# Router logits computed the other way round: the expert vectors as the stationary operand, three token tiles side by side in TensorE's columns

## What is computed

```python
# 1: linear attention, then an RMS norm           -> x [2304, 512]
# 2: dense mixture: out += p[:, e] * (relu(x @ w1[e]) @ w2[e]) for 4 experts
# 3: routed mixture, 8 experts, one for each token
xn = x / (norm(x) + 1e-6);  en = expert_emb / (norm(expert_emb) + 1e-6)
logits = xn @ en.T / tau                        # [2304, 8]
expert_idx = argmax(logits)
gate_w = softmax(logits)[expert_idx]
out[mask_e] = gate_w * (relu(x[mask_e] @ w1[e]) @ w2[e])
```

## Time and profile before

| | us |
|---|---|
| median of 3 runs | 1151.87 |
| runs | 1150.92 to 1154.58 |
| the profiled execution, own time | 1151.53 |
| its span | 1149.9 |
| PE busy | 1125.5 (98%) |
| DVE busy | 728.5 (63%) |
| ACT busy | 455.3 (40%) |
| POOL busy | 655.9 (57%) |

### The profile page before, as it was taken

The page is one execution under the profiler, slowest core; times in us unless marked ns, Lnnn a source line. Parts: engine busy times, 40 slices in busy tenths (PEclk is TensorE's granted clock), DMA queues, the critical chain, the costliest instruction groups (busy, mean ns, idle before and its releaser), DMA issues.

```text
span 1149.9 us, 18699 instructions
## 1 busy us (share of the span) xinstructions
PE 1125.5 (98%) x6206; PEld 992.3 (86%) x6207; DVE 728.5 (63%) x1159; ACT 455.3 (40%) x808; POOL 655.9 (57%) x609
## 2 busy tenths in 40 slices
PE   8999999999999999999999999999999999999996
PEld 8888889999889888998889888998887788888885
DVE  4877888888976788888875878888662222222221
ACT  4773444444434444444434444444222222222220
POOL 1587777799867777899867777777330111111101
PEclk9999999999999999999999999999989999999998
DMA  9955777777512448877612448777369749427960
GB/s 245 268 157 180 267 268 271 278 275 276 199 45 78 142 131 302 289 278 261 216 37 75 137 146 302 279 273 270 144 243 383 273 183 372 153 100 302 374 238 13
DMA packets 102433, 250.87 MB, mean 218 GB/s; under 512 B 8254, under 2 KB 48190, under 8 KB 94171
## 3 DMA queue, kind: packets, MB, share of 16 engines
q1 hardware_dynamic: 97360, 235.18, 59.2%
q0 software_dynamic: 4800, 14.72, 3.7%
q10 hardware_dynamic: 203, 0.05, 0.0%
HBM read 170.99 MB, written 79.98 MB: 218 GB/s over the span
## 4 chain that ended last, share of the span: by engine, by line
PE 82%; DVE 7%; POOL 4%; issue 3%; DMA 2%; ACT 2%; SPq 0%; DVEq 0%; POOLq 0%; ACTq 0%
PE ps L1277 25%; PE ps L1279 25%; PE ps L1278 25%; PE ps L1466 2%; DMA w_raw<-in_moe_w_dram 1%; DVE x_rows L965 1%; POOL w_lo L483 1%; PE ps L1235 1%; PE ps L1432 1%; PE ps L1370 1%; DVE hT_lo L954 1%; PE ps L1205 1%; DVE attn_rows L887 1%; DVE x_ops_lo L978 1%; DVE hT_lo L952 0%
## 5 line engine op out<-in xcount | busy, mean ns | idle before, releaser
L1277 PE MATMUL ps<-x_ops_hi,w_hi 128*128 128x384 f32 x672 | 226.5, 337 | 3.4 <-DVE sum L935 3.2
L1277 PE MATMUL ps<-w_hi,hT_hi 128*128 128x512 f32 x576 | 227.1, 394 | 0.4
L1279 PE MATMUL ps<-x_ops_hi,w_lo 128*128 128x384 f32 x672 | 225.7, 336 | 0.0
L1279 PE MATMUL ps<-w_hi,hT_lo 128*128 128x512 f32 x576 | 225.4, 391 | 0.0
L1278 PE MATMUL ps<-x_ops_lo,w_hi 128*128 128x384 f32 x672 | 225.2, 335 | 0.0
L1278 PE MATMUL ps<-w_lo,hT_hi 128*128 128x512 f32 x576 | 225.0, 391 | 0.0
L965 DVE SCALAR_TENSOR_TENSOR x_rows<-ps,dense_probs,x_rows 128x512 f32<-128x512 f32 x270 | 189.8, 738 | 22.2 <-PE ps L1279 22.2
L608 POOL DMA_INDIRECT out_dram<-y_rows,row_ids x22 | 22.6, 1026 | 237.3 <-DVE y_rows L1168 141.9
L492 POOL TENSOR_TENSOR w_lo<-w_raw,w_hi 128x512 fp32r<-128x512 f32 x96 | 149.5, 1577 | 8.0 <-ACT w_hi L702 8.0
L1158 DVE TENSOR_TENSOR rhT_lo<-ps,rhT_hi 128x512 fp32r<-128x512 f32 x44 | 28.4, 686 | 172.9 <-ACT rhT_hi L826 172.9
L478 POOL TENSOR_TENSOR w_lo<-w_raw,w_hi 128x512 fp32r<-128x512 f32 x48 | 62.2, 1295 | 126.7 <-ACT w_hi L690 126.6
(11 more groups left out here) (198 smaller groups left out, 2006.8 us busy)
## 6 DMA issues: line engine op xcount, KB each, us to landing
w_slots<-split_parts SPq DMA_DIRECT2D x64, 1024.0 KB, 5.6
w_raw<-in_moe_w_dram SPq DMA_DIRECT2D x96, 512.0 KB, 3.5
ahead_raw<-in_moe_w_dram SPq DMA_DIRECT2D x64, 512.0 KB, 6.6
split_parts<-ahead_hi SPq DMA_DIRECT2D x64, 512.0 KB, 4.4
split_parts<-ahead_lo SPq DMA_DIRECT2D x64, 512.0 KB, 5.8
row_tile<-dispatched_rows POOLq DMA_DIRECT2D x20, 257.0 KB, 5.8
kv<-in_k_dram SPq DMA_DIRECT2D x16, 288.0 KB, 7.9
kv<-in_v_dram SPq DMA_DIRECT2D x16, 288.0 KB, 8.2
```

The costliest lines, as they stand in the source:

```text
L1277: mm(out_, ah, bh, start=(first and m == 0), stop=False, skip_group_check=not final or not first)
L1279: last = mm(out_, al, bh, start=False, stop=(final and m == n - 1), skip_group_check=not final or not first)
```

## The change

For the first four blocks, `logits(t)` three times is replaced by `logits_by_tile` and `logits_by_token`. In `logits_by_tile` the expert vectors, padded with zeros to 32 columns, are stationary, and 128 transposed tokens are the moving operand; the three tiles of a block write to partitions 0, 32 and 64 of bank 3, that is to three column groups of the array. ScalarE copies the 96 x 128 result to SBUF, and `logits_by_token` brings it back to tokens on partitions with one transpose into bank 2. The first stands after `down(k - 1, 4)`, the second after `down(k - 1, 5)`. `xt` has three buffers. The last three blocks keep `logits(t)`.

```diff
+    EW = 32
...
-    enT = keep("enT", [P, KC, E2])
+    enT = keep("enT", [P, KC, EW])
...
                 act.wait_ge(xt_done, t + 1)
-                if t >= 2:
-                    act.wait_ge(lg_done, t - 1)
-                A(xt[:, t % 2, :], ps[:, t % 2, :], ACT.Copy).then_inc(xt_copied, 1)
+                if t >= 3:
+                    act.wait_ge(lg_done, t - 2)
+                A(xt[:, t % 3, :], ps[:, t % 2, :], ACT.Copy).then_inc(xt_copied, 1)
...
                         for t in range(*BLOCKS[b]):
                             route(t)
+                        act.wait_ge(lgt_done, b + 1)
+                        A(lgt[:, :], ps[0:3 * EW, 3, 0:P], ACT.Copy).then_inc(lgt_copied, 1)
...
+            V.memset(enT[:, :, :], 0.0).then_inc(enT_cleared, 1)
...
+                found = ps[:, 2, HT:HT + 3 * EW].rearrange("p (t e) -> p t e", e=EW)[:, :, 0:E2] if b in ROUTE_AT else in_bank(2, b)
+                step(V.tensor_tensor(r_("logit", b), found, wide(scl[:, slice(*BLOCKS[b])], b), ALU.mult))
...
+            def logits_by_tile(b, k):
+
+                pe.wait_ge(xt_copied, BLOCKS[b][1])
+                pe.wait_ge(c21_done, k + 1)
+                for c in range(KC):
+                    for g in range(3):
+                        last = mm(ps[g * EW:(g + 1) * EW, 3, 0:P], enT[:, c, :], xt[:, g, c * P:(c + 1) * P],
+                                  start=(c == 0), stop=(c == KC - 1))
+                last.then_inc(lgt_done, 1)
+
+            def logits_by_token(b, k):
+
+                pe.wait_ge(lgt_copied, b + 1)
+                pe.wait_ge(c12_done, k + 1)
+                if b:
+
+                    pe.wait_ge(lg_read, b)
+                tr(ps[:, 2, HT:HT + 3 * EW], lgt[:, :], ident[0:3 * EW, 0:3 * EW]).then_inc(lg_done, 3)
...
-                            if k == at_ and first <= first + j - 2 < end:
-                                logits(first + j - 2, k)
+                            if k == at_ and j == 4:
+                                logits_by_tile(b, k)
+                            if k == at_ and j == 5:
+                                logits_by_token(b, k)
                                 chosen = b + 1
```

More of the change, by code:

```diff
@@ L126, in build @@
     gi = at("gate_and_id", [P, 2, 2], F32, o + 28768)
-    xt = at("xt_route", [P, 2, D], F32, o + 28800)
-    xsq = at("route_sq", [P, D], F32, o + 32896)
+    lgt = at("logits_by_tile", [3 * EW, P], F32, o + 26464)
+    xt = at("xt_route", [P, 3, D], F32, o + 26976)
+    xsq = at("route_sq", [P, D], F32, o + 33120)
     BE = [P, BTT, E2]
@@ L138, in build @@
     cmpd = at("r_cmpd", [P, TAB, E2], F32, o + 29216)
-    assert 4 * TAB * E2 <= 960 and 4 * BTT * E2 <= 96 and 4 * E2 * TT <= 576
+    assert BTT <= 3 and 26368 + 24 * BTT <= 26464 and 4 * TAB * E2 <= 960 and 4 * BTT * E2 <= 96 and 4 * E2 * TT <= 576
     o3 = o2 + 12032
@@ L210, in build @@
         en_norm, en_step, enT_done, enT_copied = sem("en_norm"), sem("en_step"), sem("enT_done"), sem("enT_copied")
+        enT_cleared, lgt_done, lgt_copied = sem("enT_cleared"), sem("lgt_done"), sem("lgt_copied")
         p_step = sem("p_step")
@@ L912, in _ @@
             V.tensor_copy(pr[:, :, :], ps[:, 6, KC * E2:KC * E2 + E1 * TT].rearrange("p (e t) -> p t e", e=E1)).then_inc(p_step, 1)
-            V.tensor_copy(enT[:, :, :], ps[:, 6, 0:KC * E2].rearrange("p (c e) -> p c e", c=KC)).then_inc(enT_copied, 1)
+            dve.wait_ge(enT_cleared, 1)
+            V.tensor_copy(enT[:, :, 0:E2], ps[:, 6, 0:KC * E2].rearrange("p (c e) -> p c e", c=KC)).then_inc(enT_copied, 1)
             dve.wait_ge(gain_loaded, 32)
@@ L1011, in read_logits @@
                 dve.wait_ge(scaled, b + 1)
-                step(V.tensor_tensor(r_("logit", b), in_bank(2, b), wide(scl[:, slice(*BLOCKS[b])], b), ALU.mult))
+                found = ps[:, 2, HT:HT + 3 * EW].rearrange("p (t e) -> p t e", e=EW)[:, :, 0:E2] if b in ROUTE_AT else in_bank(2, b)
+                step(V.tensor_tensor(r_("logit", b), found, wide(scl[:, slice(*BLOCKS[b])], b), ALU.mult))
                 dve.sem_inc(lg_read, 1)
@@ L1369, in logits @@
                 for c in range(KC):
-                    last = mm(ps[:, 2, HT + j * E2:HT + (j + 1) * E2], xt[:, t % 2, c * P:(c + 1) * P], enT[:, c, :],
+                    last = mm(ps[:, 2, HT + j * E2:HT + (j + 1) * E2], xt[:, t % 3, c * P:(c + 1) * P], enT[:, c, 0:E2],
                               start=(c == 0), stop=(c == KC - 1))
                 last.then_inc(lg_done, 1)
+            def logits_by_tile(b, k):
[12 more added lines that the diff above has]
+                tr(ps[:, 2, HT:HT + 3 * EW], lgt[:, :], ident[0:3 * EW, 0:3 * EW]).then_inc(lg_done, 3)
             def ranks(b, k):
```

## The result

The changed kernel takes 1147.74 us (median of 8 runs, 1145.74 to 1150.23) beside 1151.41 us (median of 8 runs of the kernel before). The recorded ratio of the two is 0.9964, with a 95% interval of 0.995 to 0.9978; it is not the quotient of the medians, which is 0.9968. Forecast were 1148.3 us and a gain of 3.4 to 3.6; measured is a gain of 3.7 in the medians and of 4.1 by the ratio. A second timing of the same kernel gave 1147.55 us, 0.9962 [0.9948, 0.9976].

The account below looks back on a forecast made before the run. TensorE, busy 98% of the span, was taken as the bound; blocks give 1.37 + 0 + 1.37 + 0.70 = 3.44 us, from 1151.53 to 1148.1, in median terms 1148.4, stated as 1148.3 us, range 1146.1 to 1150.8.

Parts of the forecast that it names:

- Removed, 2.69 us a block: TensorE in each block: 3 x 4 fp32 logits matmuls, 24 load and matmul pairs at 112 ns, go away.
- Added: TensorE in each block: twelve new matmuls in three column groups, 0.91 us, mode changes 0.30, transpose 0.11; sum 1.32 us.
- The transpose: TensorE in each block: bringing the logits back to tokens on partitions costs about 0.11 us.
- Covers: `logits_by_tile` and transpose: other work hides the waits for ScalarE's copies and VectorE's additions; none of this costs anything.
- Blocks 0 and 2, -1.37 each: Steps 18 and 34: GpSimd's scale is ready before product 2, so all of 1.37 us arrives, twice, 2.74 us.
- everything follows TensorE again: Behind the waits at product 2, nothing but TensorE was taken to set the pace; no size given.
- Block 1, nothing: Step 20: the scale comes behind three scatters, so TensorE waits 1.8 us instead of 0.45 before product 2; nothing arrives.
- The rival that the new copy or the transpose held it: Posed for the experiments: block 1 gives nothing because of the new copy or transpose; no size or chance given.
- Block 3, -0.70: Step 36: GpSimd's scale ends at 660.44 and holds TensorE before product 2; of 1.37 us, 0.70 arrive.
- 1, GpSimd's end of the step moves: Scatters change: step 20 shorter 1147.1 or all four blocks 1146.0, chance 0.22; step 36 longer 1149.1, chance 0.10.
- 2, strict order: New matmuls start only in program order: 1.40 us for them, 0.88 won a block, 1149.0 to 1149.3; chance 0.14.
- 3, not side by side: `logits_by_tile`: groups run one after another, 0.35 us more a block, 1152.5 to 1152.9; chance 0.09, including similar stalls.

Follow-up runs that it names:

- logits_together: Kernel before's old logits in all four blocks, but three tiles in one piece behind `down` tile 4, with three `xt` buffers: 1156.08 us, ratio 1.0036.
- no_cover: Changed kernel with `logits_by_tile` behind j = 5, so no `down` tile lies between it and the transpose: 1150.27 us, ratio 0.9989.
- second profile: Profile of the changed kernel timed a second time, with no edit: 1147.55 us, ratio 0.9962.
- blocks_1_3: Changed kernel with the new logits in blocks 1 and 3 only, the old ones in blocks 0 and 2: 1150.32 us, ratio 0.9989.
- norms_first: Changed kernel with GpSimd's scale issued ahead of the scatters of the block before: 1146.26 us, ratio 0.9945.
- group_outer: Changed kernel with the two loops of the twelve matmuls swapped, all four of a tile before the next tile's: 1150.71 us, ratio 0.9987.
- one_group: Changed kernel with all three tiles in the same 32 columns and three transposes of 32 rows instead of one of 96: 1154.13 us, ratio 1.002.
- after: The changed kernel itself, against the kernel before: 1147.74 us, ratio 0.9964.

## Why the prediction was right, step by step

**Removed, 2.69 us a block: confirmed.** The piece in logits_together is bounded by the starts 395.45 and 398.05; with the first `down` distance behind it of 0.31 in place of 0.23 it costs 2.68.

**Added: confirmed.** In step 18 the 24 records cost from 363.65 (where the next `down` was due, 0.23 behind 363.42) to 364.74, and 0.11 more in the longer distance to 365.08: 1.20 us, forecast 0.91 + 0.30. The transpose: 0.03 in the step and 0.09 in the first distance of the next (366.27 to 366.53 in place of 0.17), forecast 0.11. The saving of PE's busy time over a pair of steps is 1.33 to 1.41, forecast 1.37. So the saving on TensorE came out as forecast term by term, and not by luck.

**Covers: confirmed.** There is no wait at L1399 while `down` tile 5 lies between; no_cover priced the cover at 0.46 us a block, and 1.08 in one of four.

**Blocks 0 and 2, -1.37 each: right in kind, 0.13 to 0.15 too small.** PE's busy time gave 1.41, and the idle time of steps 19 and 35 shrank too, from 0.12 and 0.11 to about nothing. I had taken it for granted that behind product 2 "everything follows TensorE again", which put at nothing a wait that the kernel before has in the next step. Behind `ranks`, `down` tile 5 writes the bank of tile 1, and in the program it waits until VectorE has added tile 1. From `ranks` to this `down` it took 0.42, 0.16, 0.41 and 0.44 us in steps 19, 21, 35 and 37 before, 0.34, 0.17, 0.29 and 0.17 now, and 0.16, 0.16, 0.35 and 0.16 in the second profile. The four are 0.46 us less now than before, about the 0.43 by which the sum of 3.87 is over the forecast of 3.44.

**Block 1, nothing: confirmed** by the table, by blocks_1_3 and, as to the cause, by norms_first, where only GpSimd's order is changed and the wait is gone. The rival that the new copy or the transpose held it is out: both are still there in norms_first.

**Block 3, -0.70: the mechanism right, 0.2 us too small.** At product 2 it fits: 661.71 - 639.95 = 21.76 us behind the start of step 36 before, 661.48 - 640.40 = 21.08 now, 0.68 earlier. The second matmul of the product then comes 0.08 late, and the scale was ready 20.59 us into step 36 in place of 20.49, so 0.60 arrives there. The rest comes behind that, at the `ranks` of step 37. TensorE and VectorE's addition of tile 1 before:

```profile
673.78 0.19 PE L1383 MATMUL ps<-r_oh,tri 128*128 128x24 bf16 x1
...
674.22 0.50 PE L1277 MATMUL ps<-w_hi,hT_hi 128*128 128x512 f32 x1
...
673.42 0.74 DVE L965 SCALAR_TENSOR_TENSOR x_rows<-ps,dense_probs,x_rows 128x512 f32<-128x512 f32 x1
```

and now:

```profile
673.62 0.19 PE L1410 MATMUL ps<-r_oh,tri 128*128 128x24 bf16 x1
...
673.79 0.48 PE L1285 MATMUL ps<-w_hi,hT_hi 128*128 128x512 f32 x1
...
672.48 0.74 DVE L972 SCALAR_TENSOR_TENSOR x_rows<-ps,dense_probs,x_rows 128x512 f32<-128x512 f32 x1
```

It is 0.44 us from `ranks` to the next `down` before and 0.17 now. Before, the addition ended at 674.16 and `down` tile 5 followed at 674.22; in steps 19 and 35 it followed 0.06 and 0.05 us behind the same addition. Now the addition ended at 673.22, before TensorE came: VectorE starts it 13.82 and 13.89 us into step 37, while TensorE, held up at product 2, reaches `ranks` at 15.03 where it was 14.18. That this is the wait is read from the traces and the program; no run moves VectorE's work to test it.

**Rivals.** 1, GpSimd's end of the step moves: the middle scatter of step 20 took 1.92 us as before, and that of step 36 0.96, so it did not happen by itself; norms_first is its full form and gives 1146.3 where 1146.0 was said. 2, strict order: out. It needed 1.40 us for the 24 records, and the eight rounds took 8 x 0.114 = 0.91. The clearest rows are group_outer's: tile 1's first record starts at 361.088, ahead of tile 0's sixth, seventh and eighth (361.192, 361.301 and 361.410), which stand before it in the program. The Trainium skill, "TensorE: Matmul & The Clock Gate", Part 3, has matmuls start strictly in program order; here, between column groups, these records contradict it. 3, not side by side: out for this kernel; one_group shows what it would have been, 1154.1 us with three transposes, 1152.5 to 1152.9 said for one.

The one risk that the prediction did not name is the clock. The kernel before breaks the same 24 records of 128x8 into three groups with six `down` matmuls between, and its clock holds in these steps; gathered in one piece they were followed by the lower clock in three of four places. The changed kernel puts its 24 in one piece too, and its clock holds in these steps. What makes the difference between the two pieces the runs don't show.

## What to carry to other kernels

Price a saving on the engine that bounds the kernel by the distance between starts, then ask at each place what else the next wait hangs on. Here one of four blocks gave nothing. Moving three small GpSimd operations ahead of scatters, worth next to nothing by itself, let 2.2 to 2.5 us more of the change arrive in the dense stage. Column groups pay in full only if the program alternates between them: with the groups in the outer loop 1.46 of the 3.87 us were left. Before you gather matmuls with few moving columns in one piece, look at the granted clock: here that cost it in three of four places, and the kernel became slower.

## What the runs showed of the hardware that was not expected

- A busy TensorE can lose its clock: behind 2.7 us of 128 x 128 loads with eight moving columns, and no idle time, the granted clock fell from 2.4 to 1.2 GHz in three of four places (logits_together). 24 records of 32 stationary and 128 moving columns in one piece did not do this, neither in 1.07 us (after) nor in 2.81 (one_group).
- Matmuls of one column group can start ahead of earlier ones of another: with the groups in the outer loop, tile 1's first record started beside tile 0's fifth of eight (group_outer, 1.99 us for the 24 in place of 1.07). Within a group the records stood 0.11 us apart.
- Indirect DMAs issued by GpSimd 16.97 us into step 20 took 1.30 us, then 0.97 and 0.96; issued 14.07 us into it, 1.86, 1.92 and 0.96. The trace doesn't say why.
